# Regrouped transposes, one tile loop on TensorE and running offsets for token ranks, in a fused attention, mixture-of-experts and dense MLP kernel

## What is computed

```python
# attention: batch 2, 8 heads, 768 tokens, head size 64; masked by cluster
scores = where(q_assign == k_assign, scale * q @ k.T, -1e9)
x = softmax(scores) @ v                      # 1536 tokens x 512
# mixture of experts: 8 experts, one per token
e_idx = argmax(x @ w_gate)                   # per token
for e in range(8):
    h = maximum(x[e_idx == e] @ w1[e], 0)    # 512 -> 1024
    out[e_idx == e] = gate * eom * (h @ w2[e])   # 1024 -> 512
# dense MLP, 512 -> 2048 -> 512
h = out @ w_in;  y = (h * sigmoid(1.702 * h)) @ w_out
```

## Time and profile before

| | |
|---|---|
| median of 3 runs | 801.15 us (799.76 to 804.41) |
| the profiled execution | 799.89 us, its span 798.4 us |
| mean granted clock of TensorE | 0.987 |
| busy: PE / PEld / DVE / ACT / POOL | 748.6 / 645.2 / 426.7 / 371.9 / 165.6 us |
| attention, until about | 291 us |
| expert stage, to the first dense matmul | 291 to 521 us |
| dense MLP | 521 to 798 us |

### The profile page before, as it was taken

How to read it: one execution, slowest core, us unless ns; L and a number is a source line. 1 busy time by engine, 2 the same in 40 slices (tenths; PEclk the granted TensorE clock), 3 DMA queues, 4 the chain that set the end, 5 groups by cost and what they waited for, 6 DMA issues and landing times.

```text
span 798.4 us, 11944 instructions
## 1 busy us (share of the span) xinstructions
PE 748.6 (94%) x4099; PEld 645.2 (81%) x4099; DVE 426.7 (53%) x791; ACT 371.9 (47%) x707; POOL 165.6 (21%) x253
## 2 busy tenths in 40 slices
PE   4799999999999988689999999999999999999994
PEld 3699999998999976567878787878888888888883
DVE  4678888889889856354645565463322221221221
ACT  2577877877778844454746474552111011011010
POOL 5223332332636963100101010100001000020001
PEclk9999999999999999989999999999999999999998
DMA  8684453643627345865464536060000000010001
GB/s 179 153 188 97 92 132 93 154 112 91 178 62 210 114 169 132 245 236 198 135 249 153 203 123 237 14 212 1 1 0 29 25 0 1 1 54 0 1 1 53
DMA packets 61330, 86.36 MB, mean 108 GB/s; under 512 B 32576, under 2 KB 34768, under 8 KB 60752
## 3 DMA queue, kind: packets, MB, share of 16 engines
q1 hardware_dynamic: 55728, 75.23, 33.4%
q0 software_dynamic: 3376, 6.35, 2.3%
q10 hardware_dynamic: 2160, 3.93, 1.8%
HBM read 56.01 MB, written 9.05 MB: 81 GB/s over the span
## 4 chain that ended last, share of the span: by engine, by line
PE 82%; DVE 4%; ACT 3%; issue 3%; DMA 2%; ACTq 2%; POOL 1%; SPq 1%; another core or an unknown queue 0%; DVEq 0%; POOLq 0%
PE ps L980 16%; PE ps L692 11%; PE ps L766 8%; PE ps L995 5%; PE ps L997 5%; PE ps L996 5%; PE ps L742 4%; PE ps L738 4%; PE ps L910 4%; PE ps L912 3%; PE ps L911 3%; PE ps L718 3%; PE ps L897 2%; PE ps L898 2%; PE ps L899 2%
## 5 line engine op out<-in xcount | busy, mean ns | idle before, releaser
L1240 ACT ACTIVATE g<-ps 128x512 f32<-128x512 f32 x48 | 28.7, 598 | 205.4 <-PE ps L980 205.4
L1621 DVE CAST gt_h<-g 128x512 fp32r<-128x512 f32 x48 | 20.5, 427 | 179.7 <-ACT g L1240 179.7
L1365 DVE TENSOR_TENSOR pt_l<-ps,pt_h 128x384 fp32r<-128x384 f32 x192 | 97.9, 551 | 32.5 <-ACT pt_h L1078 31.1
L1078 ACT CAST pt_h<-ps 128x384 fp32r<-128x384 f32 x192 | 84.4, 486 | 31.1 <-PE ps L692 30.9
L1330 DVE TENSOR_REDUCE nmax<-ps 128x1 f32<-128x768 f32 x96 | 90.9, 947 | 6.0 <-PE ps L742 5.9
L1055 ACT ACTIVATE probs<-ps,nmax 128x768 f32<-128x768 f32 x96 | 88.3, 920 | 6.5 <-DVE nmax L1330 6.0
L692 PE MATMUL ps<-ident,probs 128*128 128x128 f32 x576 | 83.2, 276 | 1.6 <-DVE pt_l L1365 0.7
L980 PE MATMUL ps<-x2t_h,wl 128*128 128x512 f32 x192 | 74.9, 390 | 0.3 <-DVE wl L1538 0.3
L995 PE MATMUL ps<-wh,gt_l 128*128 128x512 f32 x192 | 74.8, 390 | 0.0
L980 PE MATMUL ps<-x2t_h,wh 128*128 128x512 f32 x192 | 74.7, 389 | 0.0
L980 PE MATMUL ps<-x2t_l,wh 128*128 128x512 f32 x192 | 74.7, 389 | 0.0
(11 more groups left out here) (198 smaller groups left out, 1504.1 us busy)
## 6 DMA issues: line engine op xcount, KB each, us to landing
raw<-in_moe_w SPq DMA_DIRECT2D x32, 1024.0 KB, 7.9
ka<-hi_t SPq DMA_DIRECT2D x32, 192.0 KB
raw<-in_moe_w_in SPq DMA_DIRECT2D x4, 1024.0 KB, 6.9
raw<-in_moe_w_out SPq DMA_DIRECT2D x4, 1024.0 KB, 6.7
xg<-xs ACTq DMA_DIRECT2D x15, 256.0 KB
qn<-in_q SPq DMA_DIRECT2D x16, 192.0 KB, 3.7
kn<-in_k SPq DMA_DIRECT2D x16, 192.0 KB, 3.9
vn<-in_v SPq DMA_DIRECT2D x8, 384.0 KB, 5.2
```

Source lines behind the costliest of these rows:

```text
L1078: nc.scalar.copy(pt_h[g % 2][:, half * GT:(half + 1) * GT, t3 * P:(t3 + 1) * P], ps[:, 4 + half, 0:GQ].rearrange("p (c n) -> p c n", c=GT) ...
L1365: nc.vector.tensor_tensor(pt_l[g % 2][at_p], ps[:, 4 + half, 0:GQ].rearrange("p (c n) -> p c n", c=GT), pt_h[g % 2][at_p].bitcast(F32), AL ...
```

## The change

- `ranks`: the region start and the gap are no longer added by matmuls, and each stage counts its own tokens only. DVE keeps the running base of each stage in `offset[:, st, :]`; `place` multiplies it with the choice into a second half of `rank`, and one reduction sums both. `total` now runs in all stages and adds to `count`.
- SP: fills 0, 1 and 2 directly after the counts; `fetch_second(1)` no longer waits for `g_rows`; the loop's fill is one expert further ahead.
- POOL: the first scatter of stage 1 stands before the last `add_logits`.
- TensorE: `expert_loop(..., alike=True)` merges k = 1 and k = 2 into one loop from 1, so two copies of the tile's code per expert. The transposes stand in two pairs: the tile's with the second hidden one, the first hidden one with the output's. One more `tile_transpose` after the last tile.
- ACT: `tile_high(g + 1)` at the end of an iteration instead of `tile_high(g)` at its start behind the register loads; `turned_high(p)` before the last weight piece. DVE likewise.
- The hand-written tiles 0 and 1 follow the same order; `gate(1, ...)` of DVE moves from behind `region_rows` to directly behind the counts.

```diff
@@ expert_loop
+                if e and not alike:
                     with eng.If(n > 1):
                         tile(eng.snap(counter), e, 1)
                         eng.reg_add(counter, counter, 1)
-                with eng.If(n > 2):
-                    with eng.Fori(2, n):
+                done = 1 if e and alike else 2
+                with eng.If(n > done):
+                    with eng.Fori(done, n):
@@ SP
             sp.wait_ge(g_filled, 1)
-            fill(0)
+            for e in range(3):
+                fill(e)
             sp.wait_ge(s_pad[0], 16)
             sp.wait_ge(s_disp, 16 * NT)
             sp.dma_start(xg[:, :], xs[TILE:2 * TILE, :]).then_inc(xg_in, 16)
-            fill(1)
             sp.wait_ge(pv_done, PAIRS * NG)
-            sp.wait_ge(g_rows, 1)
             fetch_second(1)
-            fill(2)
+            fill(3)
...
-                    if e + 2 < E:
-                        fill(e + 2)
+                    if e + 3 < E:
+                        fill(e + 3)
@@ POOL
             add_logits(lastg - 1)
+            place_rows(T)
             add_logits(lastg)
@@ ranks, PE
-                nc.tensor.matmul(dst, ones[:, :], region_b[...], start=True, stop=False)
...
+                nc.tensor.matmul(dst, before[:, :], picked[:, a * E:z * E], start=True, stop=False)
+                for d in range(1, n):
+                    last = nc.tensor.matmul(dst[:, d * E:], ones[:, :], picked[:, a * E:(z - d) * E], ...)
+                last.then_inc(g_rank, 1)
+                for t in range(a, z):
+                    last = nc.tensor.matmul(total_of(st), ones[:, :], pick_b[:, t, :], ...)
+                last.then_inc(g_total, 1)
@@ PE, tiles 0 and 1
-            hidden(0, 0, 0, 0, 3)
+            hidden(0, 0, 0)
             pe.wait_ge(g_row, 2)
             ranks(2)
-            hidden(0, 0, 0, 3)
-            hidden(0, 0, 1, 0, 1)
+            hidden(0, 0, 1, 0, 2)
             hidden_transpose(0, 0)
-            hidden(0, 0, 1, 1)
+            hidden(0, 0, 1, 2)
...
+            tile_transpose(1)
             down(0, 0, 6)
-            turned(0)
-            tile_transpose(1)
             pe.wait_ge(xtl_done, 2)
             hidden(1, 0, 0)
-            hidden(1, 0, 1, 0, 1)
+            hidden(1, 0, 1, 0, 2)
             hidden_transpose(1, 0)
-            hidden(1, 0, 1, 1)
+            turned(0)
+            hidden(1, 0, 1, 2)
@@ PE, one iteration
                 down(p, ep, 0)
                 tile_transpose(g)
+                hidden_transpose(p, 1)
                 down(p, ep, 2)
-                hidden_transpose(p, 1)
                 pe.wait_ge(xtl_done, g + 1)
                 hidden(g, e, 0)
                 down(p, ep, 4)
                 down(p, ep, 6)
+                hidden(g, e, 1, 0, 2)
                 hidden_transpose(g, 0)
-                hidden(g, e, 1)
                 turned(p)
+                hidden(g, e, 1, 2)
-            expert_loop(pe, tiles, expert_tile)
+            expert_loop(pe, tiles, expert_tile, alike=True)
             down(last, E - 1, 0)
+            tile_transpose(total)
             down(last, E - 1, 2)
@@ ACT, one iteration
-                tile_high(g)
                 fetch(ahead_row, min(e + 1, E - 1))
                 high(p, 1)
-                relu(g, 0)
                 if k < 2:
                     split(whose, 0)
                     split(whose, 1)
+                relu(g, 0)
+                if k < 2:
+                    split(whose, 2)
                 scaled(p)
                 high(g, 0)
+                turned_high(p, row)
                 if k < 2:
-                    split(whose, 2)
                     split(whose, 3)
                 relu(g, 1)
-                turned_high(p, row)
+                tile_high(g + 1)
@@ DVE, behind the counts
+            gate(1, 0)
+            gate(1, 1)
             low(0, 0)
             count_tiles()
             low(0, 1)
             region_rows()
             split_first(1, 0)
-            gate(1, 0)
-            gate(1, 1)
-            turned_low(0, 0)
             tile_low(1)
```

More of the change, by code:

```diff
@@ L337, in halves, with total_of @@
             return ps[:, bank:bank + 2, 0:GQ]
+        def total_of(st):
+            return ps[:, 4, 0:E] if st else ps[:, 7, TOTAL:TOTAL + E]
         def head_of(g):
@@ L343, in score_bank, with expert_loop @@
             return 2 * (s % 2)
-        def expert_loop(eng, counter, tile, only=None):
+        def expert_loop(eng, counter, tile, only=None, alike=False):
             for e in range(E):
@@ L656, in _ @@
             add_logits(lastg - 1)
+            place_rows(T)
             add_logits(lastg)
-            for t in range(T, NT):
+            for t in range(T + 1, NT):
                 place_rows(t)
@@ L1175, in _ @@
             high(0, 0)
+            relu(0, 1)
             split_first(1, 0)
-            relu(0, 1)
             high(0, 1)
-            for i in range(1, 4):
-                split_first(1, i)
+            split_first(1, 1)
+            tile_high(1)
             scaled(0)
+            act.wait_ge(g_region, 1)
+            fetch(region_row_of(2), 1)
+            split_first(1, 2)
+            relu(1, 0)
+            high(1, 0)
             act.wait_ge(s_disp, 16 * NT)
             turned_high(0, 0)
-            tile_high(1)
-            act.wait_ge(g_region, 1)
-            fetch(region_row_of(2), 1)
-            relu(1, 0)
-            high(1, 0)
+            split_first(1, 3)
             relu(1, 1)
+            tile_high(2)
             act.wait_ge(g_tiles, 1)
@@ L1428, in total @@
             def total(st):
-                dve.wait_ge(g_total, 1 + st // 2)
-                nc.vector.tensor_copy(count[:, 1:SEG], ps[:, 7, TOTAL:TOTAL + E]).then_inc(g_count, 1)
+                dve.wait_ge(g_total, st + 1)
+                if st < 2:
+                    nc.vector.tensor_tensor(offset[:, st + 1, :], offset[:, st, :], total_of(st), ALU.add).then_inc(g_offset, 1)
+                if st:
+                    nc.vector.tensor_tensor(count[:, 1:SEG], count[:, 1:SEG], total_of(st), ALU.add).then_inc(g_count, 1)
+                else:
+                    nc.vector.tensor_copy(count[:, 1:SEG], total_of(st)).then_inc(g_count, 1)
             def place(st):
@@ L1567, in _ @@
             split_first(1, 0)
-            gate(1, 0)
-            gate(1, 1)
-            turned_low(0, 0)
             tile_low(1)
+            split_first(1, 1)
             dense_rows()
-            split_first(1, 1)
             split_first(1, 2)
             low(1, 0)
+            turned_low(0, 0)
             split_first(1, 3)
+            tile_low(2)
             dve.wait_ge(g_tiles, 1)
@@ L1591, in expert_tile @@
                 row = row_at(p + 1)
-                tile_low(g)
                 low(p, 1)
@@ L1597, in expert_tile @@
                 low(g, 0)
+                turned_low(p, row)
                 if k < 2:
@@ L1600, in expert_tile @@
                     split(whose, 3)
-                turned_low(p, row)
+                tile_low(g + 1)
             def first_of_next(e):
```

43 lines of the change are left out of this document (19 added, 24 removed).

## The result

The changed kernel takes 790.11 us (median of 4 runs, 788.40 to 792.23), the kernel before on the same chip 801.58 us: a ratio of 0.9853 (95% interval 0.9820 to 0.9886). That is faster, and inside the range of 775 to 792, but 8 us above the forecast of 782.0 and outside the narrower 776 to 786 that had a chance of 0.50. The profiled execution took 789.68 us with a span of 788.2.

What follows compares the result with a forecast made beforehand. PE was taken as the bound, 82% of the chain of waits. Tiles 0 to 3 -16.2, steady tiles -6.8, backward jump +2.0, end +1.4, attention +0.3: -19.3 us, forecast 782.0 (776 to 786; 8 in 10 from 775 to 792).

Steps and rivals of the forecast that it cites:

- Step 1: Steady tile loop: grouping transposes worth 0.0 by itself; ACT's rounding ahead of jump and loads removes xt_l waits, -6.8 us.
- Step 2: Tile 2: fills 0 to 2 ahead of the w2 transfer remove PE's 3.39 us loss and 1.7 us of low clock.
- Step 3: Expert 1 to 2: jumping one copy, not two, saves 5.1 us and 2.3 of clock; w1 pieces cost 2.7.
- Rival (a): The stall at expert 2 stays, a taken jump being a jump: +5.1 and +2.3, 789.3 us; chance 0.15.
- Step 4: PE's loop jumps back once over 138 instructions for expert 7's third tile: +2.0 us, bounds 0 and 5.3.
- Rival (d): PE's new loop fetches instructions again after each of seven passes, 5.1 us each: 815.7 us; chance 0.04.
- Step 5: Tiles 0 and 1: smaller ranks, earlier gate and reordered transposes leave 3.9 us of losses; stage starts 0.8 us earlier.
- Step 6: Behind the last tile: one more group of transposes, +0.4 us, and a later first w_in piece, +1.0; sum +1.4.
- (b): Weights become the bound in tiles 2 to 5; a late piece costs some 5 us: 787 us; chance 0.14.
- (c): The tile loop gains only half, ACT and DVE being too full: 785.4 us; chance 0.12.

Runs made afterwards that it cites:

- experiment 2: Changed kernel with SP's old order, two of the three fills back behind tile 1's load: ratio 0.9865 to the kernel before.
- experiments 11 and 12: Changed kernel with three copies of PE's tile code: ratio 0.9876 to the kernel before; the same with code shifted by 87 already-met waits: 797.88 us.
- experiment 12: Changed kernel with three copies of PE's tile code, shifted by 87 already-met waits at PE's start: 797.88 us, one run.
- experiments 3 and 4: Changed kernel with batch 1's gate late again: ratio 0.9824 to the kernel before; with only POOL's scatters held until tile 1's tokens landed: 0.9760.
- `w2` held: Changed kernel with SP's transfer of expert 1's second weights waiting until tile 1's tokens landed: 790.16 us, ratio 0.9845 to the kernel before.

## Why the prediction was right and wrong

**Step 1, transposes and roundings: size right (-5.5 to -5.7 for -6.8), account in part wrong.** The distance of steady tiles came to 12.85 us for 12.8, and PEld's waits for `xt_l` fell from 10.2 to 0.6 us. DVE's schedule "just fits", as counted. But the step said that grouping is worth 0.0 by itself. For the switch that nearly holds (0.03 us a merge; the prediction's "at most 0.02" stood there without a row). Grouping is worth 3.8 us through the order: the count of DVE's queue took `turned_low` at T + 1.9, a place it has only because `turned(p)` moved with the group. With either part undone less than a third of the gain is left. The tiles at the entries to an expert are still 0.3 to 0.6 us longer than the others (12.93 to 13.26 us for 12.66), and the wait named there is `ht_l`: ACT's `high(p, 1)` now stands behind the jump and the loads (2.35 us of "issue" ahead of it in the timeline), where `tile_high` stood before.

**Step 2, expert 2's fill: right.** No wait of ACT for a fill is left at tile 2, it comes back with SP's old order (experiment 2, 4.42 us), and the window from tile 2 to 3 is 13.6 us (324.07 to 337.66) against 26.2 before for the same section (319.53 to 345.70), which also holds step 3's stall.

**Step 3: the stall went, for a reason other than the one given.** The row of 5.11 us is gone, its clock too, and the new chain of weight pieces costs about what was forecast: tile 3 takes 16.3 us where the other first tiles of an expert take 12.9 to 13.3, so 3.0 to 3.3 us for 2.7. Its two longest waits in the changed kernel,

```profile
341.24 0.47 PE L910 MATMUL ps<-wh,xt_l 128*128 128x512 f32 x1 [1.17 <-DVE wl L1547]
...
346.05 0.51 PE L897 MATMUL ps<-wh,ht_l 128*128 128x512 f32 x1 [0.54 <-DVE ht_l L1504]
```

with the matmuls in between held back by the same pieces. "A jump over two copies cost 5.1 us, over one nothing" fell with experiments 11 and 12. Rival (a) was thus nearer than its 0.15: as far as one shift shows, the stall's absence is luck of position, and so are the 7.4 us that the step booked for it. Rival (a)'s time, 789.3, is also within 1 us of the measured one, and that is chance: its stall isn't there, and the time went to tile 0. The Trainium skill (Runtime: NRT & Kernel Launch, section "Instruction fetch mechanics") ties the price of a jump to whether its target lies in the pages at hand; experiment 12, where the same step with the code elsewhere stalls, agrees with it.

**Step 4, the backward jump: +2.0 expected, 0 measured.** PE's transposes of the last tiles in the changed kernel:

```profile
469.69 0.60 PE L696 MATMUL ps<-ident,xg 128*128 128x128 f32 x4
...
482.63 0.60 PE L696 MATMUL ps<-ident,xg 128*128 128x128 f32 x4
...
495.30 0.60 PE L696 MATMUL ps<-ident,xg 128*128 128x128 f32 x4
...
507.96 0.60 PE L696 MATMUL ps<-ident,xg 128*128 128x128 f32 x4
```

The distances are 12.94, 12.67 and 12.66 us; expert 7's third tile, the one reached by the backward jump, starts at 495.30, 12.67 behind its second. Rival (d), a fetch for each pass, is out with it. The DMA view shows no packet of instructions between 482.63 and 495.30 either. The same page and section of the Trainium skill gives TensorE 128 KiB of instruction memory, 2048 instructions, and also says that only two blocks of 256 are at hand; the 0 us agree with the first, and the estimate of 2.6 us from the second did not come, though one jump can't decide between them.

**Step 5, tiles 0 and 1: this is the step that failed.** It forecast 3.9 us of losses. In its words, `gate(1)` "takes about 1.8 us in DVE's idle time before `low(0, 0)` and frees POOL's `place_info`", and beside it stood "xg behind three fills 1.0". The working priced the gate's DVE time, the queue ahead of the load and, with 0.5 us, the scale that stands behind the scatters; that the scatters would hold up anything else it put at nothing. They are six issues that moved from 308.92 to 300.43, into the load of tile 1 and the hidden value of tile 0. Held, they give back 7.0 us; the changed kernel's 790.1 less that is 783.1, one us off the forecast. By sections: 59.0 us from tile 0 to 4, 13.5 less than before for 16.2 expected, with 1.8 us for tile 2's load and 1.3 us for a hidden value still lost. The fills, which the step priced at 1.0, don't hold the load up by themselves (2.8 us from issue to landing in experiments 3 and 4). The step's gain of 0.8 us at the ranks came: tile 0's first `hidden` starts 3.33 us behind its transposes (288.40 to 291.73) for 4.23 before.

**Step 6, behind the last tile: right**, +1.0 to +1.2 for +1.4. The wait of 0.33 us at the dense MLP's second group is 1.36 us.

**Rivals.** (b), weights as the bound: no row of a wait for a weight transfer appeared. (c), half the loop's gain: out at 12.85 us a tile, but with either part of step 1 left out not even half would have come.

**The version that beats both.** The changed kernel with the scatters held runs at 0.9760 (0.9727 to 0.9793) of the kernel before, against 0.9853 (0.9820 to 0.9886) for the change as made.

## What to carry to other kernels

When a step is moved forward, list every issue that waits for it on every queue, and look at what is on its way at the new time; here the gate's own step hardly showed (the kernel with the scatters held keeps it and meets the forecast within 1 us), and the early scatters cost 2.6 us on one chip and 7.0 on another. Before counting a stall as a gain, ask what runs under it: the same stall was worth 1.3 us in one order and some 6 us in the other. And two reorderings whose gains pass through one full queue have to be tried together, since with one of them undone 1.3 or 1.7 of 5.5 us were left.

## What was not expected of the hardware

Six scatters of 128 rows of two numbers each delay what is beside them by far more than their bytes. On the chips at 797 us the 256 KB load took 5.0 to 6.9 us from issue to landing in place of 2.8 with the scatters out of its way; in the longest case the DMA engines reached 300 GB/s 6.0 us behind its issue, in the other 1.8 us behind it. On another kind of chip the delay showed in ACT's rows as waits of 4.47 and 5.63 us for PE's results with no releaser found, 3.09 us and none with the scatters held. In three profiles with early scatters on chips where the kernel before takes 801 us it had this form (the changed kernel, `w2` held, the shifted code), and in none of the profiles on the chips at 797 us. The Trainium skill (DMA: Bandwidth & Descriptors, section "Queues, rings and completion order") has each DMA engine go round its queues packet by packet; an estimate from that page is that some 770 small rows on 16 engines would hold up a load by a few packets, and the 2.2 to 4.1 us measured speak against it as the whole account. What in the chip the two forms have in common was not tested: neither fewer scatters, nor wider rows, nor another target were tried.

The stall of a jump hangs, as far as two profiles on two chips show, on the place of the code: 4.32 us with a shift of 87 waits, none without, the rest of the program being the same. In each stall one packet of instructions (0.02 MB) is on its way.
